# A mixture-of-experts kernel: the first slot's order of weight splits, and the place of the last overflow table

## What is computed

```python
def _moe_ref(x, w_skip, w_gate, w1, w2):
    do_compute = (x @ w_skip) > 0          # the other rows stay as they are
    xc = x[do_compute]
    logits = xc @ w_gate
    e_idx = np.argmax(logits, axis=1)
    # gate_w: the softmax weight of the chosen expert
    for e in range(E):
        mask = e_idx == e
        h = np.maximum(xc[mask] @ w1[e], 0.0)
        y[mask] = gate_w[mask, None] * (h @ w2[e])
    out[do_compute] = xc + y

def _moe2_ref(x, expert_emb, tau, w1, w2):
    logits = (x / norm(x)) @ (expert_emb / norm(expert_emb)).T / tau
    expert_idx = np.argmax(logits, axis=1)
    for e in range(E):
        mask = expert_idx == e
        h = np.maximum(x[mask] @ w1[e], 0.0)
        out[mask] = gate_w[mask, None] * (h @ w2[e])
```

## Time and profile before

| | us |
|---|---|
| median of 3 runs | 813.38 (813.21 to 814.14) |
| the profiled execution, whole | 813.1 |
| its span, first to last instruction | 811.3 |
| TensorE busy with matmuls, of the span | 674.3 |
| VectorE busy | 655.7 |
| ScalarE busy | 480.1 |

### The profile page before, as it was taken

How to read it: one execution, slowest core, us unless ns; L and a number is a source line. 1 busy time by engine, 2 the same in 40 slices (tenths; PEclk the granted TensorE clock), 3 DMA queues, 4 the chain that set the end, 5 groups by cost and what they waited for, 6 DMA issues and landing times.

```text
span 811.3 us, 17899 instructions
## 1 busy us (share of the span) xinstructions
PE 674.3 (83%) x6792; PEld 630.3 (78%) x6792; DVE 655.7 (81%) x1241; ACT 480.1 (59%) x673; POOL 213.5 (26%) x183
## 2 busy tenths in 40 slices
PE   0634342089999999938999999999999999999997
PEld 0413231088888888928999999999999989999997
DVE  7998999989999999966868667756898687676572
ACT  7688898567766666453656555545644544554541
POOL 3200000011111111013343456632344332233422
PEclk9765655589999999969999999999999999999999
DMA  7221311018833333455765665667665755665640
GB/s 190 60 71 44 88 44 29 0 51 146 173 118 107 116 95 109 138 105 192 246 226 181 222 207 192 223 197 243 209 200 186 257 187 197 223 225 188 233 151 30
DMA packets 78342, 123.77 MB, mean 153 GB/s; under 512 B 12986, under 2 KB 60582, under 8 KB 78096
## 3 DMA queue, kind: packets, MB, share of 16 engines
q1 hardware_dynamic: 71120, 106.43, 43.2%
q0 software_dynamic: 7168, 16.64, 5.8%
HBM read 111.30 MB, written 13.75 MB: 154 GB/s over the span
## 4 chain that ended last, share of the span: by engine, by line
PE 46%; DVE 6%; DMA 2%; issue 1%; ACT 1%; POOL 0%; POOLq 0%; SPq 0%; DVEq 0%
PE banks L1281 20%; PE banks L1345 14%; PE banks L1328 8%; PE banks L1256 2%; DVE w_lo L899 2%; PE banks L1266 1%; DMA raw<-w1b 1%; DMA raw<-w1a 1%; DVE mix_spot L1544 1%; DVE mix_hT_lo L1643 1%; PE banks L1263 1%; DVE w_lo L905 1%; ACT w_hi L889 0%; DMA xbuf<-mix_y,to_scatter 0%; DVE mix_y L1667 0%
## 5 line engine op out<-in xcount | busy, mean ns | idle before, releaser
L1281 PE MATMUL banks<-mix_xT_hi,w_hi 128*128 128x240 f32 x576 | 159.8, 277 | 0.6 <-DVE mix_xT_lo L1652 0.6
L1281 PE MATMUL banks<-mix_xT_lo,w_hi 128*128 128x240 f32 x576 | 159.2, 276 | 0.0
L1281 PE MATMUL banks<-mix_xT_hi,w_lo 128*128 128x240 f32 x576 | 158.0, 274 | 0.0
L709 PE MATMUL banks<-sq,ident 128*128 128x288 f32 x104 | 49.7, 662 | 81.4 <-ACT sq L626 81.4
L1382 ACT ACTIVATE mix_hT_hi<-banks 128x480 fp32r<-128x480 f32 x96 | 54.8, 572 | 105.6 <-PE banks L1281 103.2
L1281 PEld LDWEIGHTS banks<-mix_xT_hi,w_hi 128*128 128x128 f32 x576 | 108.9, 189 | 0.9 <-issue 0.8
L1281 PEld LDWEIGHTS banks<-mix_xT_hi,w_lo 128*128 128x128 f32 x576 | 109.4, 190 | 0.0
L1281 PEld LDWEIGHTS banks<-mix_xT_lo,w_hi 128*128 128x128 f32 x576 | 109.2, 190 | 0.0
L709 PEld LDWEIGHTS banks<-sq,ident 128*128 128x128 f32 x104 | 32.7, 325 | 97.2 <-ACT sq L626 62.8
L1643 DVE SCALAR_TENSOR_TENSOR mix_hT_lo<-banks,mix_hT_hi 128x480 fp32r<-128x480 f32 x96 | 62.7, 653 | 55.7 <-ACT mix_hT_hi L1382 53.6
L1345 PE MATMUL banks<-w_hi,mix_hT_hi 128*128 128x384 f32 (+1 forms) x256 | 89.8, 351 | 1.5 <-DVE mix_hT_lo L1643 1.5
(11 more groups left out here) (236 smaller groups left out, 1696.9 us busy)
## 6 DMA issues: line engine op xcount, KB each, us to landing
raw<-w1b SPq DMA_DIRECT2D x16, 1536.0 KB, 7.8
raw<-w2b SPq DMA_DIRECT2D x16, 1536.0 KB, 6.7
raw<-w1a SPq DMA_DIRECT2D x8, 1536.0 KB
raw<-w2a SPq DMA_DIRECT2D x8, 1536.0 KB, 7.8
ring<-a SPq DMA_DIRECT2D x9, 864.0 KB, 4.9
qk<-q SPq DMA_DIRECT2D x48, 96.0 KB, 2.3
qk<-k SPq DMA_DIRECT2D x48, 96.0 KB, 2.3
vt<-v SPq DMA_DIRECT2D x24, 192.0 KB, 2.5
```

Source lines behind the costliest of these rows:

```text
L709: last = pe.matmul(banks[:, c, 0:STEP * PSEG].rearrange("p (t s) -> p t s", t=STEP), ident[:, :], sq[:, c * STEP:(c + 1) * STEP, j, :], st ...
L1281: last = pe.matmul(pU[g % TURNS][:, n * N:(n + 1) * N], w1p[m][:, b, c, f * P:(f + 1) * P], xT[s][:, c, 0:N], start=(c == 0 and (s, m) == ...
```

## The change

Three edits, all of order.

1. Slot `(0, 0)`, VectorE: both `lo_part2` of the slot's own second weights go from behind `hidden(0)` and `hidden(1)` to the end of the head, directly behind the split of the rows.
2. Slot `(0, 0)`: ScalarE casts the next slot's first weights behind `hidden(2)` and `hidden(3)` instead of behind `hidden(0)` and `hidden(1)`; VectorE makes their low parts behind `hidden(3)`.
3. Slot `(1, 7)`: VectorE's `over_entries` of phase 2 goes from ahead of the next weights' low parts to behind `hidden(3)`, and TensorE's four chunks of `list_over` go from blocks 1 to 4 of half 0 to blocks 4 to 7 of half 1.

```diff
@@ list_part, by_token (TensorE)
-                    if (ph.n, slot.at) == (1, 7):
-                        list_over(phases[2], units)
...
                         if half == 0:
                             list_part(ph, slot, f)
+                        elif (ph.n, slot.at) == (1, 7) and f >= FC // 2:
+                            list_over(phases[2], range((f - FC // 2) * CHUNK, (f - FC // 2 + 1) * CHUNK))
@@ body (ScalarE)
                 hidden(slot, 0)
-                if nxt is not None:
+                if nxt is not None and (ph.n, slot.at) != (0, 0):
                     weights.hi_part1(act, nxt, 0)
                 hidden(slot, 1)
-                if nxt is not None:
+                if nxt is not None and (ph.n, slot.at) != (0, 0):
                     weights.hi_part1(act, nxt, 1)
...
+                if (ph.n, slot.at) == (0, 0):
+                    weights.hi_part1(act, nxt, 0)
                 hidden(slot, 3)
+                if (ph.n, slot.at) == (0, 0):
+                    weights.hi_part1(act, nxt, 1)
@@ body (VectorE)
                 hidden(slot, 0)
                 if before is not None:
                     finish(before, oldest, 0)
-                if at == (0, 0):
-                    weights.lo_part2(dve, slot, 0)
                 hidden(slot, 1)
                 if before is not None:
                     finish(before, oldest, 1)
-                if at == (0, 0):
-                    weights.lo_part2(dve, slot, 1)
...
+                if nxt is not None and at != (0, 0):
+                    weights.lo_part1(dve, nxt, 0)
+                hidden(slot, 2)
+                if nxt is not None and at != (0, 0):
+                    weights.lo_part1(dve, nxt, 1)
+                hidden(slot, 3)
                 if at == (1, 7):
                     over_entries(phases[2])
-                if nxt is not None:
+                if at == (0, 0):
                     weights.lo_part1(dve, nxt, 0)
-                hidden(slot, 2)
-                if nxt is not None:
                     weights.lo_part1(dve, nxt, 1)
-                hidden(slot, 3)
@@ the head (VectorE)
             gates(head.ph)
             total(head.ph)
+            for half in range(2):
+                weights.lo_part2(dve, head, half)
```

## The result

| | before | after |
|---|---|---|
| median of the runs, us | 813.76 (813.21 to 814.57, 4 runs) | 807.38 (807.12 to 808.19, 4 runs) |
| profiled execution, us | 813.1 | 807.12 |
| its span, us | 811.3 | 805.4 |

The ratio is 0.9923 [0.9905, 0.994]: 6.3 us faster [4.9, 7.7], where 3.7 was predicted and 809.0 to 811.3 was the range. Measured again it was 0.9937 [0.9924, 0.9949], 5.1 us [4.2, 6.2]. So the direction was right and the size was not: both medians of the changed kernel, 807.38 and 808.78, lie under the range. The first figure is likely 1.2 us too large by the luck of a comparison of four runs. The step from 3.7 to 5.1 is what the experiments look for.

The account below looks back on a forecast made before the run. TensorE's chain of matmuls was taken to bound the kernel's second part, so only its pauses counted: 2.2 + 1.5 = 3.7 us off, 809.4 from the profiled 813.1, or 809.7 on the median, as predicted; range 809.0 to 811.3.

Parts of the forecast that it names:

- the term was 1.5: Slot (1, 7), second product: moving the last overflow table behind the fourth activation saves 1.5 us, lower bound 0.93.
- Gain here: First slot: TensorE begins the second product at 378.24 instead of 380.48, taken as 2.2 us, bounds 2.1 and 2.24.
- Half a us of spread between runs: Whole kernel: allowance for scatter between runs, set beside bounds adding to 3.0 and 3.75 for the range 809.0 to 810.6.
- after the routing has begun: Where TensorE's remaining waits were placed: 2.1 us for second weights, 0.7 for overflow entries, 1.5 for low activations.
- rival 1: Slot (1, 7): the late table makes TensorE wait in the second half, only the first slot pays; 811.2 us, chance 0.09.
- rival 2: First slot: another wait takes the pause's place, so only the last part pays; 811.9 us, chance 0.07.
- rival 3: Passage between the phases: scatter and load set the time, both gains are given back; 813.4 us, chance 0.04.
- Rival 4: First slot, ScalarE's cast: the early second-weights load holds back the first weights; slower, 814.6 us for landing at 387, chance 0.03.

## Why the prediction was right, and where it was wrong

*Right: the mechanism of both parts.* The view of waits lost its entries of L905 and L1614. In the first slot the pause between the products went: 8.23 us from start to start instead of 10.47 in the first pair of traces, 2.2 us as the term had it. Slot (1, 7) went from 12.0 to 12.2 us down to 10.5, 1.6 us; the term was 1.5. Margins held: low activation 0, forecast for 3.6 us behind the first product's start, stands 3.55 us behind it, the table was ready before TensorE came, and its reader at 664.67 held nobody up.

*Wrong: the step "Gain here" of the first slot*, 2.2 us with bounds 2.1 and 2.24. It took the length of the pause in one execution for what the pause costs; the runs show 3.5 in its place. Three things were missing:

- The pause's length isn't fixed. It ends on a load that took 7.5 to 8.0 us and was issued 0.9 to 1.8 us ahead of the first product. The view of waits has 1.9 to 2.7 us in six traces, mean 2.3. From start to start, as the term was counted, it is 10.6 us between the products on average, 2.5 more than without the pause.
- TensorE's clock falls behind it in three of six traces, at 1.6 us each: 0.8 on average. Filling the pause won 0.9. The term put this at nothing.
- The late subtraction also releases the buffer of the second weights late: TensorE waited 0.2 us and 0.9 us for what followed in two traces, 0.2 on average of the six. The text weighed what the earlier load might cost and never what the late one did cost.

Together 2.5 + 0.8 + 0.2 = 3.5 us, as the traces have it in one piece; the timed runs gave 4.3 [3.3, 5.3] for this part alone. With the table's 1.6 that makes 5.1 beside 5.1 [4.2, 6.2]. This sum is worked out after the fact, its 0.2 rests on two traces, and a match to the tenth is luck, with 0.3 of doubt in the mean of the six.

*Wrong: the width.* "Half a us of spread between runs" was read from three runs. The unchanged kernel spreads over 811.2 to 815.5 in twelve, for the start of the recurrence alone moves everything behind it by 2.4 us. With four runs on a side that was good for another 1.2 us here. The sentence that a trace's span may be moved onto the median by its 0.3 us was empty for the same reason: the span carries that execution's own start.

*Wrong in the wording, not in the sum:* the waits "after the routing has begun". They are the ones from the first slot on. The whole list has two longer ones within the routing itself, at 352 us (4.0) and 358 us (5.1), which the change leaves as they are.

*The rivals.* Rivals 1, 2 and 3 fell with the two parts seen in the traces; rival 1 by ten traces against four, though the timed runs of the table alone gave no more than 0.7 [-0.2, 1.5]. Rival 4, the slow one, did not come. The load of the first weights, with that of the second issued 5.05 us behind it, took 7.6 us to land, as in the earlier trace rows; the second took 8.5. The Trainium skill, "DMA: Bandwidth & Descriptors", section "Queues, rings and completion order", has one ring's descriptors taken in order, and this pair of loads agrees with it: the one behind paid, and nothing waited for it.

*Open:* what decides whether the clock falls behind a pause of 2 us; whether the timed runs of the table alone are low, and those of the first slot alone high, by chance.

## What to carry to other kernels

Price a pause of TensorE by what stands behind it too: look at the granted clock and at the time of the same matmuls just after it, in more than one execution, and at the transfers that the late work releases. Before a difference of half a per cent is explained, run the unchanged kernel a dozen times and find the instruction at which its executions part. Two edits that each break the same chain of waits are worth one of them.

## What the runs showed of the hardware

- A pause of 1.9 to 2.7 us of TensorE was followed by a granted clock of 0.50 (1.2 GHz) in three of six traces, for about 16 matmuls at 0.21 instead of 0.11 us, and by no fall in the other three. In one of the three, followed matmul by matmul, it fell 1.2 us after TensorE was busy again. With 18 small matmuls in the pause it stayed at 1.00 in the one trace taken, and in the six traces without a pause too.
- The first matmuls after 22 us of standing still cost a different amount each time: twelve of them 4.57 to 6.10 us, 3.18 with 150 turns of the unit matrix ahead of them. This alone explains most of the 2.4 us by which executions of one kernel part.
- Two loads of 1536 KB at a distance of 5.05 us on one queue took 7.6 and 8.5 us.
